# Layer 2's last tile: second products in two halves of 256 tokens

## What is computed

```python
def _moe_ref(x, w_in, w_out):
    h = x @ w_in                                 # 3072 x 2048
    g = np.where(h >= 1, h, np.where(h <= -1, 0.0, (h + 1) ** 2 / 4.0))
    return (g @ w_out).astype(np.float32)        # 3072 x 384

def _moe2_ref(x, w_in, w_out):
    h = x @ w_in
    r = np.maximum(h, 0.0)
    return ((r * r) @ w_out).astype(np.float32)
```

## Time and profile before

| | |
|---|---|
| median of 3 runs | 976.78 us (976.59 to 978.29) |
| profiled execution, first to last instruction | 975.8 us |
| PE busy | 962.4 us (99%) |
| PEld busy | 781.8 us (80%) |
| DVE busy | 601.0 us (62%) |
| ACT busy | 430.9 us (44%) |
| a step of layer 2 | 18 matmuls |
| last stores | 3 DMAs of 256 KB |

### The profile page before, as it was taken

How to read it: one execution, slowest core, us unless ns; L and a number is a source line. 1 busy time by engine, 2 the same in 40 slices (tenths; PEclk the granted TensorE clock), 3 DMA queues, 4 the chain that set the end, 5 groups by cost and what they waited for, 6 DMA issues and landing times.

```text
span 975.8 us, 22918 instructions
## 1 busy us (share of the span) xinstructions
PE 962.4 (99%) x9520; PEld 781.8 (80%) x9520; DVE 601.0 (62%) x1480; ACT 430.9 (44%) x735; POOL 42.0 (4%) x59
## 2 busy tenths in 40 slices
PE   8899999999999999999999999999999999999998
PEld 7688788777877877787778888888888888888887
DVE  7789888787978787889647763434334334333332
ACT  6667543453455435544545553333333333333333
POOL 5810000000000000000000000000000000000000
PEclk9999999999999999999999999999999999999999
DMA  8252131113012201110004411010010010000000
GB/s 261 81 174 67 59 119 48 27 38 91 35 34 73 71 21 33 49 55 2 2 20 155 162 33 65 1 65 1 1 65 1 0 65 1 33 1 1 33 1 32
DMA packets 28838, 50.65 MB, mean 52 GB/s; under 512 B 2368, under 2 KB 17728, under 8 KB 28736
## 3 DMA queue, kind: packets, MB, share of 16 engines
q1 hardware_dynamic: 28736, 49.19, 15.4%
HBM read 39.75 MB, written 9.44 MB: 50 GB/s over the span
## 4 chain that ended last, share of the span: by engine, by line
PE 87%; DVE 5%; ACT 5%; DMA 2%; issue 1%; SPq 1%; DVEq 0%; ACTq 0%
PE psum L1354 37%; PE psum L1330 37%; PE psum L1077 2%; PE psum L1163 2%; PE psum L1102 1%; PE psum L1214 1%; DVE act_g L1659 1%; ACT kn_sb L804 1%; PE psum L1221 1%; DMA ring<-in_v_s 1%; PE psum L1028 1%; PE psum L1246 1%; ACT act_g L890 1%; DVE diag L1476 1%; ACT u_sb L814 1%
## 5 line engine op out<-in xcount | busy, mean ns | idle before, releaser
L1330 PE MATMUL psum<-x_hi,w 128*128 128x512 f32 x1152 | 390.1, 394 | 0.0
L1354 PE MATMUL psum<-g_hi,w 128*128 128x512 f32 x1152 | 389.7, 393 | 0.0
L1330 PEld LDWEIGHTS psum<-x_hi,w 128*128 128x128 f32 x1152 | 216.1, 188 | 48.9
L1354 PEld LDWEIGHTS psum<-g_hi,w 128*128 128x128 f32 x1152 | 216.1, 188 | 48.4 <-issue 1.8
L1665 DVE TENSOR_TENSOR g_lo<-act_g,g_hi 128x512 fp32r<-128x512 f32 x192 | 132.3, 689 | 159.7 <-ACT g_hi L903 158.6
L1354 PE MATMUL psum<-g_lo,w 128*128 128x512 f32 x576 | 224.3, 389 | 0.0
L903 ACT ACTIVATE g_hi<-act_g 128x512 fp32r<-128x512 f32 x192 | 121.3, 632 | 232.8 <-PE psum L1354 170.6
L1330 PE MATMUL psum<-x_lo,w 128*128 128x512 f32 x576 | 224.0, 389 | 0.0
L1659 DVE TENSOR_TENSOR act_g<-act_g 128x512 f32<-128x512 f32 x96 | 66.4, 691 | 112.1 <-ACT act_g L896 112.1
L1354 PEld LDWEIGHTS psum<-g_lo,w 128*128 128x128 f32 x576 | 108.2, 188 | 21.4
L1330 PEld LDWEIGHTS psum<-x_lo,w 128*128 128x128 f32 x576 | 108.2, 188 | 21.3
(11 more groups left out here) (148 smaller groups left out, 622.0 us busy)
## 6 DMA issues: line engine op xcount, KB each, us to landing
kt_sb<-in_k_t SPq DMA_DIRECT2D x24, 256.0 KB, 4.2
qt_sb<-in_q_t SPq DMA_DIRECT2D x23, 256.0 KB, 3.3
ring<-in_v_s SPq DMA_DIRECT2D x24, 192.0 KB, 3.0
between_layers<-y_out SPq DMA_DIRECT2D x6, 768.0 KB, 4.4
x_sb<-between_layers SPq DMA_DIRECT2D x6, 768.0 KB, 5.6
result<-y_out SPq DMA_DIRECT2D x5, 768.0 KB, 3.9
gram_or_states<-in_k_s SPq DMA_DIRECT2D x15, 192.0 KB, 2.4
wi_st<-in_w_in SPq DMA_DIRECT2D x7, 384.0 KB, 3.6
```

The lines of the kernel that those rows point to most:

```text
L1330: ins = pe.matmul(h_ps[n % 2][:, :], w_in_part(layer, f // GW, part)[:, kt, fs], x[:, kt, :], start=(at == 0), stop=(at == len(terms) - 1))
L1354: ins = pe.matmul(acc[kt][:, :], w_out_part(layer, f // GW, part)[:, f % GW, ds], g[n % 2][:, :], start=(f == 0 and j == 0), stop=(f == NF ...
```

## The change

For t = 5 of layer 2 alone, `second_product` runs its nine matmuls over tokens 0 to 255 of the tile and then again over tokens 256 to 511. The first half adds to columns 0 to 255 of banks 2 to 4 and the second half to columns 0 to 255 of banks 5 to 7. Since banks 5 to 7 hold tile 4 until ScalarE has copied them, TensorE waits at f = 0 for `acc_ready` of all tile 4's copies. The weight block is loaded again for each half, so a step has 18 second-product matmuls of 256 columns with 18 loads in place of 9 of 512 with 9 loads. At the end ScalarE makes six copies of [128, 256] and SyncE six stores of [128, 256], 1 KB in a row, in the order half 0 kt 0 to 2, half 1 kt 0 to 2.

```diff
+HT = TT // 2
...
+        def last_acc(part):
+
+            return [bank[:, 0:HT] for bank in acc_ps[part]]
...
-            for kt in range(KT):
-                sp.wait_ge(acc_ready, KT * (2 * NTT - 1) + kt + 1)
-                sp.dma_start(out.rearrange("(k p) (t j) -> t p k j", p=P, j=TT)[NTT - 1][:, kt, :], y_out[:, kt, :]
-                             ).then_inc(out_stored, 16)
-            sp.wait_ge(out_stored, 16 * (2 * NTT - 1 + KT))
+            for part in range(2):
+                times = slice(part * HT, (part + 1) * HT)
+                for kt in range(KT):
+                    sp.wait_ge(acc_ready, KT * (2 * NTT - 1) + part * KT + kt + 1)
+                    sp.dma_start(out.rearrange("(k p) (t j) -> t p k j", p=P, j=TT)[NTT - 1][:, kt, times], y_out[:, kt, times]
+                                 ).then_inc(out_stored, 16)
+            sp.wait_ge(out_stored, 16 * (2 * NTT - 1 + 2 * KT))
...
+                if layer and t == NTT - 1:
+                    for part in range(2):
+                        times = slice(part * HT, (part + 1) * HT)
+                        for kt in range(KT):
+                            act.wait_ge(tail_done, part * KT + kt + 1)
+                            act.activation(y_out[:, kt, times], last_acc(part)[kt], ACT.Copy).then_inc(acc_ready, 1)
+                    return
                 for kt in range(KT):
-                    if layer and t == NTT - 1:
-                        act.wait_ge(tail_done, kt + 1)
                     act.activation(y_out[:, kt, :], acc_of(layer, t)[kt][:, :], ACT.Copy).then_inc(acc_ready, 1)
...
+                if layer and t == NTT - 1:
+                    if f == 0:
+                        pe.wait_ge(acc_ready, KT * (NTT + t))
+                    for half_of in range(2):
+                        times = slice(half_of * HT, (half_of + 1) * HT)
+                        for kt in range(KT):
+                            ds = slice(kt * P, (kt + 1) * P)
+                            for j, (part, g) in enumerate(((HIGH, g_hi), (HIGH, g_lo), (LOW, g_hi))):
+                                ins = pe.matmul(last_acc(half_of)[kt], w_out_part(layer, f // GW, part)[:, f % GW, ds],
+                                                g[n % 2][:, times], start=(f == 0 and j == 0), stop=(f == NF - 1 and j == 2))
+                            if f == NF - 1:
+                                ins.then_inc(tail_done, 1)
+                    if f < NF - 1:
+                        ins.then_inc(mm2_done, 1)
+                    return
```

## The result

| | before | changed |
|---|---|---|
| median | 976.72 us (976.16 to 978.29, 5 runs) | 980.62 us (978.93 to 981.13, 5 runs) |
| ratio | | 1.0032, 95% interval 1.0021 to 1.0043 |
| profiled execution, first to last instruction | 975.8 us | 978.9 us |
| its last tile, from the relu of its first step to the end | 70.36 us | 73.31 us |

The changed kernel is slower by some 3 us. The ratio and its interval (2.1 to 4.2 us) are the record's estimate over all these runs; the quotient of the two medians is 1.0040. The forecast was 977.8 us, within 0.2% of before; the measured time lies above its range.

What follows compares the result with a forecast made beforehand. The prediction took TensorE to bound the kernel; its terms, 0.48 + 0.35 + 0.2 = +1.0 us, took 976.78 to 977.8 us, ratio 1.001, counted as the same. The range was 976.6 to 979.5.

Steps and rivals of the forecast that it cites:

- What bounds the kernel: TensorE, busy 99% of the span and without slack in the last tile, so delays there aren't given back.
- Term 1: At tile 5's first second product TensorE waits for tile 4's copies: +0.48 us, bounds 0.32 to 0.65.
- Term 2: In the last tile's halved second products a 256-column matmul costs 0.1146 us, not 0.1133: +0.35 us, bounds -1.2 to +1.8.
- first rival: Float32r's surplus is a fixed price per matmul: 256 columns cost 120.0 ns, term 2 is +1.8, time 979.3; chance 0.20.
- The weight loads: The doubled loads in the last tile's second products stay hidden and cost nothing, at a cover of 5 ns.
- Term 3: At the end, SyncE issues six stores some 0.475 us apart and bounds the finish: +0.2 us, lower bounds -0.2 and -0.5.
- third rival: At the end SyncE keeps up and the last copy's shortening shows: -0.5 there, time 977.1; chance 0.09.
- The base: The median of the runs stands 1.0 us above the profiled span, so a span of 976.8 became 977.8.

Runs made afterwards that it cites:

- the wait alone: The kernel before, with only TensorE's wait for tile 4's three copies added at tile 5's first second product: 977.85 us against 977.28, ratio 1.0003.
- every other step: The kernel before, with tile 5's second products in two halves of 256 columns only at odd f, same banks: 979.68 us against 977.17.

## Why the prediction was wrong

**What bounds the kernel**: right. TensorE without slack; each cost on it came out in full at the end.

**Term 1, the wait**: right in mechanism, 0.57 us (the wait alone) against 0.48. Two parts were undersized. The release took 0.12 from the copy's end to the load, where the rows at 309 us gave 0.06, and the eight matmuls behind the first cost 0.04 more, which the term had at nothing. Moved behind the first half, it is gone but for 0.05.

**Term 2, the price of 256 columns**: this is the step that failed. The working had both answers, 114.6 and 120.0 ns, and chose by "a stream that reads half as much has half as much to stumble over". That was no row. The split of the surplus (11 ns inside the stream, 2.5 between) looked like evidence for it but wasn't. The profile's ends of matmuls are modelled, and here each end stands 0.16 us behind the next matmul's start, whatever the length: 389 - 227 = 162 ns for 512 columns, 283 - 120 = 163 for 256, 0.47 - 0.31 = 0.16 for the stalled one. So a duration says nothing more than the distance between two starts, and not where in a matmul the time goes. The "nothing left over" of plain float32 was a rounding: 592 - 163 = 429 ns and not 427, so some 2 ns were left. What the runs showed instead is a surplus of 13.3 ns for each matmul of 256 to 512 columns. The measured 0.120 makes a second product 0.113 longer, fifteen of them +1.7 us, where the term had +0.35. The first rival, with this price at a chance of 0.20, was the case that came. (The 118.3 ns from which it was to count as slower is a slip: 272 x 0.0050 is 1.36 and not 1.3, so 1.95 us is reached at 118.0. Nothing hangs on it.)

**What no term had**: the 512-column matmuls behind a run of narrow ones run slower for one product: 13 first products x 0.027 = +0.35 us. The prediction put this at nothing without a reason. The runs show where it comes from (every other step), and that a stall does the same, not why.

**The weight loads**: right to cost them at nothing, and by a narrow margin. With 192 and 128 columns a matmul costs 0.112 us, which is put down to its load. The cover at 256 columns is 8 ns; at 192 columns it is gone.

**Term 3, the end**: SyncE as the bound was right, with issues 0.476 apart on average as the earlier trace rows gave. From second product 191's start to the end: 978.90 - 973.25 = 5.65 us against 975.79 - 970.51 = 5.28, so +0.37 where I had +0.2; the landing, 1.8 and not 1.7, and a sixth issue that came 0.03 later in its place than forecast are the rest. The third rival was wrong about its size: without SyncE's queue it would have met the data 0.12 us on.

**The sum**: 0.57 + 1.7 + 0.35 + 0.37 = 3.0, against 2.95 in the stretch.

**The base**: the median of before was set 1.0 us above the span. But a run's time is 1.7 to 1.8 us above its own span in all runs but one (980.62 and 978.9, 978.95 and 977.2, 976.39 and 974.6; the single run of every other step has 979.68 and 977.3). The 1.0 had put one execution's span beside other executions' median. This cost the prediction nothing in itself, since the sum is a difference, but the medians of before, 976.7 to 977.6 from set to set, scatter by as much as the whole term 1, and the first comparison had 0.9 us of this on top of the 2.95.

**The range** ended at 979.5, little over the first rival's 979.3. That rival with the two things it lacked (0.35 for the first products and the 0.26 by which terms 1 and 3 were low), and with 1.7 for its 1.8, is 979.8, and the measured 980.6 holds the scatter besides. A top that is meant to hold a rival has to hold its error too.

## What to carry to other kernels

Cutting a matmul's columns in two isn't free on TensorE even when the weight loads stay hidden: for float32r with a 128x128 weight block each matmul cost its columns at 2.4 GHz plus 13 ns, with a floor of 0.112 us. Only the steps whose result is needed early should be cut. Here that is the last step alone: every other step mixes whole and halved second products in the same three banks, so the accumulation doesn't ask for the cut in all 16. No run cuts only the last step, or has ScalarE copy one half of a bank while TensorE adds to the other, so what that would gain is open. Before a transfer's last piece is shortened, look whether the pieces stream without a gap; then only starting the first one earlier can help. And where a price isn't in the trace and the sum's verdict hangs on it, a plausible scaling is no reason to give one bound three times the other's chance.

## What the hardware showed that I had not expected

- float32r, 128x128 weights, clock 1.00: 0.227 us for 512 columns, 0.173 for 384 once settled, 0.147 for 320, 0.120 for 256, and 0.112 for both 192 and 128.
- After eighteen 256-column matmuls the next nine of 512 took 2.07 us and not 2.04; after the cut at 384 it was 2.14. Behind the cut at 256 it was 2.04 again one product later. The first 384-column matmuls behind 512 were slow too, up to 0.185 for 0.173.
- The price of a matmul came one matmul late: the first of 128 columns cost 0.06 and the first of 512 behind it 0.28, and for 256 columns these were 0.114 and 0.233.
- Nine matmuls of 512 columns behind a stall of TensorE had gaps of up to 0.236, with no narrow matmul near.
- Six stores of 128 KB that SyncE issues 0.476 apart land 1.7 to 1.8 us after their issue, those of 256 KB 2.0: half the bytes save 0.2 to 0.3 us of 2.0.
- Stores with 1 KB rows streamed at 385 GB/s, those with 2 KB rows at 394 to 410.
